# Experts in fixed pairs, each on half of the array's columns

## The chip, the cores and the metric

One core of a Trainium2 chip runs the whole program in one launch. The metric is the device time of a run in microseconds. A profiled execution gives the trace; it has a span (first to last instruction) and a time of its own.

## The reference

Three parts follow one another, all in float32. `_attn_ref`: attention over a window of 128 keys for 4 batches, 8 heads, 576 positions, head size 64. Its output is laid out as 2304 tokens of 512. `_moe_ref`: a mixture of experts over these tokens. `_moe2_ref`: a feed-forward part of width 2048. What matters here is the middle one, with E = 8, D = 512, F = 1024:

```python
do_compute = (x @ w_skip) > 0            # the other tokens stay as they are
xc = x[do_compute]
logits = xc @ w_gate
e_idx = np.argmax(logits, axis=1)
gate_w = softmax(logits)[e_idx]          # per token
for e in range(E):
    mask = e_idx == e
    h = np.maximum(xc[mask] @ w1[e], 0.0)
    y[mask] = gate_w[mask, None] * (h @ w2[e])
out[do_compute] = xc + y
```

Each expert's weights are two matrices of 2 MB. With the inputs as the reference draws them, 1015 of 2304 tokens are computed, and the experts get 102, 111, 174, 146, 175, 133, 94 and 80 of them.

## The kernel before

`program` runs three blocks: `attention`, `experts`, `feed_forward`. A block ends with a barrier of all engines.

**Attention.** 16 pairs of heads (`PAIRS`) are worked off in turn. SP's queue, in the loop over n (L232 to L248), loads v of the next pair, q and k of the one after, one sixteenth of the feed-forward's weights into `ffn["raw"]` (`load_weights`, 512 KB), and stores five tiles of the pair before into the DRAM tensor `tokens`. In `times_values` (L503) the two heads of a pair write partitions 0 to 63 and 64 to 127 of the same PSUM tile.

**Experts.** First the routing, on VectorE with some matmuls. A job is 128 rows of one expert. Each expert has as many jobs as its tokens fill chunks of 128 (L820 to L827), the table says for each job and row which token it holds (`what`, `at_row`, L840 to L846, and the matmuls of L915), and `job_e_i` names the expert of each job. The register `total` is the number of jobs; an engine runs `one(j, slot)` for two jobs and then, in `later_jobs` (L640), under `If`, for those that exist. In a job:

- GpSimd copies the row list (L687), gathers 128 tokens into `x_in` (L691) and, when y is there, scatters it back (L699, L704). A gather of job j + 1 comes behind the scatter of job j - 1.
- PE transposes the tokens (`transpose_x`, L926), multiplies by w1 (`hidden`, L936, two halves c of 512 columns in four steps each; a record in the trace is half of an fp32 matmul, so 16 records), transposes relu(h) (`transpose_h`, L942) and multiplies by w2 (`output`, L952, 16 records).
- VectorE takes relu (L864) and scales y (L885). y lies in the second half of `h_sb`, so relu of the second half waits for the scatter of the job before. ScalarE copies the transposes to SBUF (L742, L750, L757).

SP loads an expert's two matrices into one of two slots when the jobs of the expert two before it are done and the next gather has landed (L666 to L672). In the block's start the first expert is loaded beside the routing. In the first two jobs the weights of the feed-forward are split for the fp32r multiplications: ScalarE copies each of 16 pieces from `raw` to `hi` (L737), VectorE subtracts `lo = raw - hi` (L872); `lo` has the place of `raw`.

**Feed-forward.** Six chunks of 384 tokens in 16 steps f each; its first matmuls wait for all pieces of `lo` (L1264).

`keep_warm` (L73) is a run of matmuls without use in the routing.

Of the kernel before, what the change touches and what calls it, by code (L numbers as in the profile page):

```python
# [8 lines left out]

# [7 lines left out]
F32 = mybir.dt.float32  # L17
F32R = mybir.dt.float32r
I32 = mybir.dt.int32
# [22 lines left out]
FILL = 240  # L42
# [3 lines left out]
CH = N // P  # L46
JOBS = CH + E
# [38 lines left out]
def attention(nc, ctx, dram, ffn, cst):  # L86
# [106 lines left out]
    def _(sp):  # L193
# [23 lines left out]

        def store(n, i):
# [13 lines left out]
        for n in range(PAIRS):  # L232
# [10 lines left out]
            load_weights(n)  # L243
# [297 lines left out]
def experts(nc, ctx, dram, ffn, cst):  # L541
# [9 lines left out]
    w1_sb = sb("w1_sb", [P, 2 * KD * F1])  # L551
    w2_sb = sb("w2_sb", [P, 2 * FB * D])
# [3 lines left out]
    x_in = sb("x_in", [P, 2, D])  # L556
# [3 lines left out]
    used = [FB * D]  # L560

    def scratch(width):
        used[0] += width
        return w2_sb[:, used[0] - width:used[0]]
# [7 lines left out]
    rank, row, weight, number, job1 = (scratch(TT) for _ in range(5))  # L572
# [8 lines left out]
    by_expert = scratch(E * E).rearrange("p (a b) -> p a b", a=E)  # L581
    passed = scratch(JOBS * E).rearrange("p (a b) -> p a b", a=JOBS)
    chunks, ends, first1 = (scratch(E) for _ in range(3))
    job_e = scratch(JOBS)
    count_i = sb("count_i", [P, E], I32)
    ends_i = sb("ends_i", [1, E], I32)
    job_e_i = sb("job_e_i", [1, JOBS + 6], I32)
    table = sb("table", [P, JOBS + 6, 2], I32)
    job_entry = sb("job_entry", [P, 2, 2], I32)
    scatter_list = sb("scatter_list", [P, 2], I32)  # L590
# [19 lines left out]
    w1_loaded = sem("w1_loaded")  # L610
    w2_loaded = sem("w2_loaded")
    entry_copied = sem("entry_copied")
    list_copied = sem("list_copied")
    gathered = sem("gathered")
    xt_ready = sem("xt_ready")
    xt_copied = sem("xt_copied")
    h_ready = sem("h_ready")
    h_relu = sem("h_relu")
    ht_ready = sem("ht_ready")
    ht_copied = sem("ht_copied")  # L620
    y_ready = sem("y_ready")
    y_scaled = sem("y_scaled")
    y_scattered = sem("y_scattered")
    block = ctx.enter_context(nc.Block())

    tables = w1_sb[:, KD * F1:KD * F1 + sum(TABLES.values())]
# [4 lines left out]
    at_row = w1_sb[:, KD * F1 + at:KD * F1 + at + TT * P].rearrange("p (t r) -> p t r", t=TT)  # L631
# [4 lines left out]
    def count_jobs(eng):  # L636
        eng.wait_ge(jobs_ready, 1)
        return eng.value_load(ends_i[0:1, E - 1:E], min_val=E, max_val=JOBS)

    def later_jobs(eng, total, pair, behind=0):  # L640


        with eng.Fori(2, JOBS, 6) as start:
# [5 lines left out]
    def _(sp):  # L649
        sp.dma_start(tables, dram["tables"]).then_inc(tables_loaded, 16)  # L650

        def load_expert(e, slot):
            sp.dma_start(w1_sb[:, slot * KD * F1:(slot + 1) * KD * F1].rearrange("p (k f) -> p k f", k=KD),
                         dram["w1"][e].rearrange("(k p) f -> p k f", p=P)).then_inc(w1_loaded, 16)
            if e:
                sp.wait_ge(w2_loaded, 16 * e)
            sp.dma_start(w2_sb[:, slot * F1 * KD:(slot + 1) * F1 * KD].rearrange("p (k f) -> p k f", f=D),
                         dram["w2"][e].rearrange("(k p) f -> p k f", p=P)).then_inc(w2_loaded, 16)
            sp.wait_ge(w1_loaded, 16 * (e + 1))

        load_expert(0, 0)

        sp.wait_ge(gathered, 32)
        load_expert(1, 1)
        sp.wait_ge(jobs_ready, 1)
        for e in range(2, E):  # L666

            end = sp.value_load(ends_i[0:1, e - 2:e - 1], min_val=1, max_val=JOBS)
            sp.wait_ge(y_ready, end)

            sp.wait_ge(gathered, end * 16 + 32)
            load_expert(e, e % 2)  # L672

    @block.gpsimd
    def _(pool):
        pool.wait_ge(table_ready, 1)
        total = count_jobs(pool)

        def gather(j, slot, later):
            if later:  # L680
                pool.wait_ge(list_copied, j - 1)
                pool.wait_ge(y_scaled, j - 1)
                settled(pool, cst)
            if not isinstance(j, int) or j:
                pool.wait_ge(gathered, j * 16)
                settled(pool, cst)
            nc.gpsimd.tensor_copy(job_entry[:, slot, :], table[:, bass.ds(j, 1), :].rearrange(  # L687
                "p o k -> p (o k)")).then_inc(entry_copied, 1)
            pool.wait_ge(entry_copied, j + 1)
            settled(pool, cst)  # L690
            nc.gpsimd.indirect_dma_start(x_in[:, slot, :], None, dram["x"],  # L691
                                         bass.IndirectOffsetOnAxis(job_entry[:, slot, 0:1], 0),
                                         bounds_check=N + P - 1, oob_is_err=False).then_inc(gathered, 16)

        def scatter(j, slot, later=True):
            if later:
                pool.wait_ge(y_scattered, (j - 1) * 16)
            settled(pool, cst)
            nc.gpsimd.tensor_copy(scatter_list[:, slot:slot + 1], job_entry[:, slot, 0:1]).then_inc(list_copied, 1)  # L699
            pool.wait_ge(list_copied, j + 1)  # L700
            settled(pool, cst)
            pool.wait_ge(y_scaled, j + 1)
            settled(pool, cst)
            nc.gpsimd.indirect_dma_start(dram["x"], bass.IndirectOffsetOnAxis(scatter_list[:, slot:slot + 1], 0),  # L704
                                         y_sb, None, bounds_check=N - 1,
                                         oob_is_err=False).then_inc(y_scattered, 16)


        gather(0, 0, False)
        gather(1, 1, False)  # L710
        scatter(0, 0, False)

        def pair(first):
            with pool.If(first < total):
                gather(first, 0, True)
            with pool.If(first - 1 < total):
                scatter(first - 1, 1)
            with pool.If(first + 1 < total):
                gather(first + 1, 1, True)
            with pool.If(first < total):  # L720
                scatter(first, 0)

        later_jobs(pool, total, pair, behind=1)
        with pool.If(total > JOBS - 1):
            scatter(JOBS - 1, 1)

        pool.wait_ge(y_scattered, total * 16)

    @block.scalar
    def _(act):  # L730
# [3 lines left out]
        act.wait_ge(cst["w_loaded"], 16 * PAIRS)  # L734
        for n in range(PAIRS):
            piece = slice(n * 1024, n * 1024 + 1024)
# [624 lines left out]
```

## Time and profile before

| | us |
|---|---|
| median of three runs | 836.48 (835.88 to 838.04) |
| time of the profiled execution | 835.62 |
| its span | 833.8 |
| attention, up to the routing's first instruction | 178 |
| routing, up to the first transposes of a job | 178 to 202 |
| twelve jobs | 202 to 392 |
| feed-forward, from its first load | 399 to 834 |

The engines' busy times in the span are 796.8 us for PE (96%), 495.9 for VectorE, 367.4 for ScalarE and 357.9 for GpSimd; the mean granted clock of TensorE is 0.99 of full speed. Read a job by the starts on PE's timeline, not by the busy times: the records of a pipelined matmul overlap.

### The profile page before, as it was taken

To read this page: it belongs to the slowest core of one execution; us is meant where nothing else is said; L and a number is where in the kernel's file an instruction comes from. 1 tells how busy PE (TensorE), PEld (TensorE's weight loads), DVE (VectorE), ACT (ScalarE), POOL (GpSimd) and SP (SyncE) were. 2 spreads that over 40 slices of the span, in tenths; PEclk is the share of its full clock that TensorE was granted. 3 is DMA by queue.
4 is the path that set the end of the run, shared out by engine and by line. 5 is a ranking of instruction groups with operands and counts; after the bars stand their busy time and mean duration, and the time that the engine had idled before them with its cause. 6 is when DMAs were issued, how large, how long until landed. Compare 5 with 4: busy or idle time off the path is not lost.

```text
span 833.8 us, 14016 instructions
## 1 busy us (share of the span) xinstructions
PE 796.8 (96%) x4436; PEld 614.5 (74%) x4437; DVE 495.9 (59%) x876; ACT 367.4 (44%) x881; POOL 357.9 (43%) x455
## 2 busy tenths in 40 slices
PE   8999999998999999997599999999999999999996
PEld 4788788876444444443588888888888888988995
DVE  3666666663641111111478877878786887787784
ACT  4677676635110110100355455554555455446453
POOL 3555555301111111111156655655565565655564
PEclk9999999999999999999799999999999999999999
DMA  5656556643584633633200110110100010000001
GB/s 197 190 166 166 165 166 171 164 162 106 216 303 150 243 104 141 240 115 116 75 1 1 39 39 1 38 39 1 39 0 38 0 38 38 0 0 22 18 1 38
DMA packets 50626, 78.07 MB, mean 94 GB/s; under 512 B 22275, under 2 KB 23555, under 8 KB 50560
## 3 DMA queue, kind: packets, MB, share of 16 engines
q1 hardware_dynamic: 48656, 72.20, 26.3%
q0 software_dynamic: 1920, 5.23, 2.0%
q8 instruction: 28, 0.46, 0.2%
q14 instruction: 22, 0.18, 0.1%
HBM read 65.90 MB, written 12.85 MB: 94 GB/s over the span
## 4 chain that ended last, share of the span: by engine, by line
PE 45%; DVE 2%; issue 2%; ACT 1%; POOL 1%; DMA 0%; POOLq 0%; ACTq 0%; DVEq 0%
PE ffn_o L1248 22%; PE ffn_h L1235 22%; DVE n_sb L1206 1%; PE ffn_xt L1223 1%; POOL n_sb L1111 1%; ACT r_sb L1156 1%; DVE u_sb L1189 0%; ACT o_sb L1168 0%; POOL g_lo L1117 0%; DVE u_sb L1198 0%; DVE n_sb L1193 0%; DMA x_sb<-tokens 0%; DVE xt_lo L1180 0%; PE ffn_o L1268 0%; ACT r_sb L1158 0%
## 5 line engine op out<-in xcount | busy, mean ns | idle before, releaser
L1117 POOL TENSOR_TENSOR g_lo<-n_sb,g_hi 128x384 fp32r<-128x384 f32 x96 | 120.0, 1250 | 174.0 <-ACT g_hi L1151 172.0
L1235 PE MATMUL ffn_h<-xt_hi,ffn_lo 128*128 128x384 f32 x384 | 131.4, 342 | 1.9 <-DVE xt_lo L1180 1.9
L1111 POOL TENSOR_TENSOR n_sb<-n_sb,r_sb 128x384 f32<-128x384 f32 x96 | 125.4, 1307 | 18.2 <-DVE r_sb L1200 18.2
L1156 ACT ACTIVATE r_sb<-n_sb,all_consts 128x384 f32<-128x384 f32 x96 | 59.3, 617 | 163.3 <-DVE n_sb L1206 163.3
L1235 PE MATMUL ffn_h<-xt_lo,ffn_hi 128*128 128x384 f32 x384 | 129.7, 338 | 0.0
L1235 PE MATMUL ffn_h<-xt_hi,ffn_hi 128*128 128x384 f32 x384 | 129.1, 336 | 0.0
L1206 DVE SCALAR_TENSOR_TENSOR n_sb<-u_sb 128x384 f32<-128x384 f32 x96 | 124.8, 1300 | 1.8 <-ACT u_sb L1145 1.8
L1248 PE MATMUL ffn_o<-ffn_hi,g_lo 128*128 128x512 f32 x288 | 115.5, 401 | 10.4 <-POOL g_lo L1117 5.3
L1248 PE MATMUL ffn_o<-ffn_hi,g_hi 128*128 128x512 f32 x288 | 113.8, 395 | 0.0
L1248 PE MATMUL ffn_o<-ffn_lo,g_hi 128*128 128x512 f32 x288 | 113.4, 394 | 0.0
L936 PE MATMUL ps_h<-w_sb,x_t 128*128 x192 | 86.3, 603 | 1.1 <-ACT x_t L742 0.9
L1189 DVE TENSOR_SCALAR u_sb<-ffn_h 128x384 f32<-128x384 f32 x96 | 53.2, 554 | 47.2 <-PE ffn_h L1235 47.0
L335 ACT ACTIVATE probs<-ps_scores,neg_max 128x256 f32<-128x256 f32 (+2 forms) x160 | 66.8, 427 | 29.5 <-DVE neg_max L376 29.5
L704 POOL DMA_INDIRECT tokens<-h_sb,scatter_list x12 | 12.2, 1020 | 154.7 <-DVE h_sb L885 154.7
L750 ACT ACTIVATE h_t<-ps_ht 128x512 f32<-128x512 f32 x12 | 7.2, 598 | 159.0 <-PE ps_ht L942 159.0
L1235 PEld LDWEIGHTS ffn_h<-xt_hi,ffn_lo 128*128 128x128 f32 x384 | 72.4, 188 | 5.2 <-DVE xt_lo L1180 2.3
L1235 PEld LDWEIGHTS ffn_h<-xt_lo,ffn_hi 128*128 128x128 f32 x384 | 72.4, 188 | 3.2
L936 PEld LDWEIGHTS ps_h<-w_sb,x_t 128*128 128x128 f32 x192 | 36.9, 194 | 48.4 <-issue 48.4
L1248 PEld LDWEIGHTS ffn_o<-ffn_hi,g_lo 128*128 128x128 f32 x288 | 54.1, 188 | 24.9 <-issue 11.2
L1235 PEld LDWEIGHTS ffn_h<-xt_hi,ffn_hi 128*128 128x128 f32 x384 | 72.3, 188 | 0.0
L1145 ACT ACTIVATE u_sb<-u_sb 128x384 f32<-128x384 f32 x96 | 50.1, 522 | 38.0 <-DVE u_sb L1189 37.8
L376 DVE TENSOR_REDUCE neg_max<-ps_scores 128x2 f32<-128x512 f32 (+2 forms) x80 | 43.6, 578 | 36.5 <-PE ps_scores L475 35.9
(138 smaller groups left out, 1368.4 us busy)
## 6 DMA issues: line engine op xcount, KB each, us to landing
w_sb<-in_w SPq DMA_DIRECT2D x16, 2048.0 KB, 7.9
ffn_raw<-in_w_ffn SPq DMA_DIRECT2D x16, 512.0 KB, 5.3
q_raw<-in_qT SPq DMA_DIRECT2D x16, 288.0 KB, 3.9
k_raw<-in_kT SPq DMA_DIRECT2D x16, 288.0 KB, 4.1
v_sb<-in_v SPq DMA_DIRECT2D x16, 256.0 KB, 2.6
tokens<-x_out SPq DMA_DIRECT2D x64, 64.0 KB, 3.2
x_sb<-tokens SPq DMA_DIRECT2D x5, 768.0 KB, 4.5
out<-o_sb SPq DMA_DIRECT2D x5, 768.0 KB, 3.6
```

The lines of the kernel that those rows point to most:

```text
L335: e = nc.scalar.activation(probs[0:n, r, h, 0:w], ps_scores[t.ring][0:n, h, 0:w], ACT.Exp, bias=neg_max[0:n, r, h:h + 1], scale=-1.0, accu ...
L376: nc.vector.tensor_reduce(neg_max[0:n, r], ps_scores[t.ring][0:n, :, 0:w], AX_X, ALU.min).then_inc(max_ready, 1)
L704: nc.gpsimd.indirect_dma_start(dram["x"], bass.IndirectOffsetOnAxis(scatter_list[:, slot:slot + 1], 0), y_sb, None, bounds_check=N - 1, oo ...
L936: m = t_.matmul(ps_h[c][:, :], x_t[:, k, :], w, start=(k == 0), stop=(k == KD - 1))
L1111: nc.gpsimd.tensor_tensor(n_sb[:, f % NB], n_sb[:, f % NB], r_sb[:, f % 2], ALU.mult).then_inc(ratio_ready, 1)
L1117: nc.gpsimd.tensor_tensor(g_lo[:, f % 2], n_sb[:, f % NB], g_hi[:, f % 2].bitcast(F32), ALU.subtract).then_inc(g_lo_ready, 1)
L1145: nc.scalar.activation(u_sb[:, t.r], u_sb[:, t.r], ACT.Exp).then_inc(u_ready, 1)
L1156: nc.scalar.activation(r_sb[:, t.r], n_sb[:, t.f % NB], ACT.Ln, bias=cst["two"]).then_inc(ln_ready, 1)
L1189: v.tensor_scalar(u_sb[:, t.r], ps_h[t.f % HB][:, 0:C], 20.0, None, ALU.min).then_inc(min_ready, 1)
L1206: v.scalar_tensor_tensor(out=n_sb[:, t.f % NB], in0=u_sb[:, t.r], scalar=2.0, in1=u_sb[:, t.r], op0=ALU.add, op1=ALU.mult).then_inc(n_read ...
L1235: m = nc.tensor.matmul(ps_h[t.f % HB][:, 0:C], ffn[a][:, at:at + P], b[:, t.par, k], start=(n == 0), stop=(n == 3 * KD - 1))
L1248: m = nc.tensor.matmul(ps_o[i][:, :], a[:, t.r, P * i:P * i + P], ffn[b][:, at:at + D], start=(t.f == 0 and n == 0), stop=(t.f == FT - 1 a ...
```

## The change

The eight experts form four fixed pairs (0, 1), (2, 3), (4, 5), (6, 7), worked off in four phases p. A job has 64 rows for each expert of the pair: rows 0 to 63 hold tokens of the even one, rows 64 to 127 of the odd one (`side` adds 64 to the row). A phase has as many jobs as the larger of the two has chunks of 64, at least one. Every matmul of `hidden` and `output` becomes two, with 64 columns of weights each (here the tokens are the stationary operand, the expert's matrix streams), which write partitions 0 to 63 and 64 to 127. The transposes stay as they were. All addresses of weights are fixed in a phase; each engine loads only the number of jobs at its start, and has its own loop for later jobs in each phase.

A pair's weights are 8 MB. Even pairs lie where `hi` will be (`experts_even`), odd ones in `w_sb`, whose space the routing uses before. Pair 0 is loaded in the attention in four loads at n = 6, 8, 10, 12. Pair 1 is loaded when the first gathers have landed, pairs 2 and 3 when the jobs of the pair two before are done; SP doesn't wait for gathers any more. Each phase has semaphores of its own. GpSimd gathers the first two tiles of pair p + 1 before it scatters the first job of pair p; PE transposes the first of them within that job, and ScalarE copies it to `x_first`.

The split of the feed-forward's weights moves: 14 of the 16 pieces are split in the last phase, four of their subtractions on GpSimd; the last two pieces, where `x_in` lies now, are loaded at the feed-forward's start and split in steps 5 and 7 of its first chunk. `FILL` goes from 240 to 216 columns, because the constants have fewer columns.

```diff
-FILL = 240
+FILL = 216
+POOL_PIECES = 4
+LATE = 2
+EARLY = PAIRS - LATE
 TT = B * QT
 GE = E + 1
-CH = N // P
-JOBS = CH + E
+W = P // 2
+PH = E // 2
+PHASE = N // W
+JOBS = PHASE + PH - 1
+LOG_W = W.bit_length() - 1
...
+def pair_weights(dram, buffer, p):
+    first = 2 * KD * F1
+    for half in range(2):
+        yield (buffer[:, half * KD * F1:(half + 1) * KD * F1].rearrange("p (k f) -> p k f", k=KD),
+               dram["w1"][2 * p + half].rearrange("(k p) f -> p k f", p=P))
+    for half in range(2):
+        yield (buffer[:, first + half * KD * F1:first + (half + 1) * KD * F1].rearrange("p (k f) -> p k f", f=D),
+               dram["w2"][2 * p + half].rearrange("(k p) f -> p k f", p=P))
...
+            if n < EARLY:
+                load_weights(n)
+            if n >= HP + 2 and n % 2 == 0 and n < HP + 10:
+                load_experts((n - HP - 2) // 2)
...
-        def load_expert(e, slot):
...
+        def load_experts(p):
+            for i, (to, of) in enumerate(pair_weights(dram, pairs[p % 2], p)):
+                if i == 2:
+                    sp.wait_ge(w1_loaded[p], 32)
+                sp.dma_start(to, of).then_inc(w1_loaded[p] if i < 2 else w2_loaded[p], 16)
+        sp.wait_ge(first_gathered, 1)
+        load_experts(1)
         sp.wait_ge(jobs_ready, 1)
-        for e in range(2, E):
-            end = sp.value_load(ends_i[0:1, e - 2:e - 1], min_val=1, max_val=JOBS)
-            sp.wait_ge(y_ready, end)
-            sp.wait_ge(gathered, end * 16 + 32)
-            load_expert(e, e % 2)
+        for p in range(2, PH):
+            done = jobs_of(sp, p - 2)
+            sp.wait_ge(y_ready[p - 2], done)
+            settled(sp, cst)
+            load_experts(p)
...
+        def gather_two(p):
+            total = jobs_of(pool, p)
+            first = pool.value_load(jobs_i[0:1, PH + p:PH + p + 1], min_val=0, max_val=JOBS - 1) if p else 0
+            gather(p, 0, 0, first)
+            with pool.If(total > 1):
+                gather(p, 1, 1, first)
+                if p == 0:
+                    pool.wait_ge(gathered[0], 32)
+            if p == 0:
+                pool.wait_ge(gathered[0], 16)
+                pool.sem_inc(first_gathered, 1)
+            return total, first
+        def low_parts():
+            for n in range(POOL_PIECES):
+                piece = slice(n * 1024, n * 1024 + 1024)
+                pool.wait_ge(cst["w_hi_ready"], n + 1)
+                nc.gpsimd.tensor_tensor(ffn["lo"][:, piece], ffn["raw"][:, piece], ffn["hi"][:, piece].bitcast(F32),
+                                        ALU.subtract).then_inc(cst["w_lo_by_pool"], 1)
...
+        ahead, before = gather_two(0), None
+        for p in range(PH):
+            total, first = ahead
+            if p < PH - 1:
+                ahead = gather_two(p + 1)
+            else:
+                low_parts()
+            scatter(p, 0, 0, before)
...
+            if p == PH - 1:
+                act.wait_ge(cst["w_loaded"], 16 * EARLY)
+                act.wait_ge(y_ready[p - 1], before)
+                high_parts(range(7))
+            one_now = functools.partial(one, p, total=total)
+            one_now(0, 0)
+            if p == PH - 1:
+                high_parts(range(7, EARLY))
...
+        then(v.tensor_tensor(in_job[:, :, 0:E], onehot, over_t(cst["odd"]), ALU.mult))
+        then(v.tensor_reduce(side, in_job[:, :, 0:E], AX_X, ALU.add))
...
+            split = p == PH - 1 and isinstance(i, int) and i == 0
+            relu(p, i, 0, before)
+            if split:
+                low_parts(range(4, 5))
+            relu(p, i, 1, before)
+            if split:
+                low_parts(range(5, 11))
+            scale_y(p, i, slot)
+            if split:
+                low_parts(range(11, 13))
...
-                m = t_.matmul(ps_h[c][:, :], x_t[:, k, :], w, start=(k == 0), stop=(k == KD - 1))
...
+        def hidden(p, i, c):
+            x = x_t
+            if isinstance(i, int) and i == 0:
+                x = x_first
+                if c == 0:
+                    pe.wait_ge(first_copied, p + 1)
+                    pe.wait_ge(w1_loaded[p], 32)
+            elif c == 0:
+                pe.wait_ge(xt_copied[p], i)
+            for k in range(KD):
+                for side in range(2):
+                    mine = slice(W * side, W * side + W)
+                    m = t_.matmul(ps_h[c][mine, :], x[:, k, mine], weights(p, 0, side, k * F1 + c * half),
+                                  start=(k == 0), stop=(k == KD - 1))
+            m.then_inc(h_ready[p], 1)
...
+        def one(p, i, slot, total, done_before=None):
+            hidden(p, i, 0)
+            hidden(p, i, 1)
+            transpose_h(p, i, 0)
+            with pe.If(i + 1 < total):
+                transpose_x(p, i + 1, 1 - slot)
+            if isinstance(i, int) and i == 0 and p < PH - 1:
+                transpose_first(p + 1)
+            transpose_h(p, i, 1)
+            if not isinstance(i, int):
+                pe.wait_ge(y_scaled[p], i - 1)
+            elif i == 0 and p:
+                pe.wait_ge(y_scaled[p - 1], done_before)
+            output(p, i, slot, 0)
+            output(p, i, slot, 1)
...
+        for n in range(EARLY, PAIRS):
+            sp.dma_start(ffn["raw"][:, n * 1024:n * 1024 + 1024], dram["w_ffn"][n]).then_inc(cst["w_loaded"], 16)
...
+            if isinstance(c, int) and c == 0 and f in SPLIT:
+                piece = slice(SPLIT[f] * 1024, SPLIT[f] * 1024 + 1024)
+                act.wait_ge(cst["w_loaded"], 16 * PAIRS)
+                nc.scalar.activation(ffn["hi"][:, piece], ffn["raw"][:, piece],
+                                     ACT.Copy).then_inc(cst["w_hi_ready"], 1)
...
+            if isinstance(t.c, int) and t.c == 0 and t.f == FT - 2 * LATE:
+                pe.wait_ge(cst["w_lo_ready"], PAIRS - POOL_PIECES)
...
+        ffn["pair"] = nc.alloc_sbuf_tensor_at("experts_even", [P, 4 * KD * F1], F32, offset=ffn["free"])
+        ffn["late"] = at_lo + EARLY * 1024 * 4
```

`output` is split like `hidden`, `scatter` and `gather` only take the phase beside the job, and `relu` waits for the scatter before it also across two phases.

## Rows read from the trace of the kernel before

**Rows 1.** Windows: length, PE, PEld, DVE, ACT, POOL busy, clock, DMA share, GB/s.

```profile
280.00:320.00 40.00, 39.83 (x111) 18.76 (x110) 5.71 (x8) 3.37 (x6) 7.38 (x12) 1.00 0.58 210
...
418.00:421.00 3.00, 3.00 (x12) 2.56 (x11) 2.65 (x4) 1.20 (x4) 2.00 (x2) 0.51 0.00 0
```

**Rows 2.** Timeline of PE, jobs of the expert stage, first feed-forward `output`.

```profile
236.93 7.13 PE L936 MATMUL ps_h<-w_sb,x_t 128*128 x16
243.90 0.60 PE L942 MATMUL ps_ht<-all_consts,h_sb 128*128 128x128 f32 x4
244.33 0.61 PE L926 MATMUL ps_xt<-all_consts,x_in 128*128 128x128 f32 x4
244.94 0.66 PE L942 MATMUL ps_ht<-all_consts,h_sb 128*128 128x128 f32 x4
245.44 3.60 PE L952 MATMUL ps_y<-w_sb,h_t 128*128 x8
...
252.31 7.03 PE L936 MATMUL ps_h<-w_sb,x_t 128*128 x16
...
360.46 7.03 PE L936 MATMUL ps_h<-w_sb,x_t 128*128 x16
...
416.62 0.47 PE L1248 MATMUL ffn_o<-ffn_hi,g_lo 128*128 128x512 f32 x1 [1.89 <-POOL g_lo L1117]
```

**Rows 3.** Timeline of SP's queue, loads of experts 3 and 4.

```profile
244.26 0.38 SPq L653 DMA_DIRECT2D w_sb<-in_w  x1
...
275.53 0.37 SPq L653 DMA_DIRECT2D w_sb<-in_w  x1
```

**Rows 4.** Timeline of PE in the attention; last, line 503 (ns min/median/max).

```profile
110.90 0.22 PE L475 MATMUL ps_scores<-k_hi,q_lo 64*64 64x64 f32 x2
110.95 0.22 PE L475 MATMUL ps_scores<-k_hi,q_hi 64*64 64x64 f32 x2
...
111.50 1.09 PE L503 MATMUL ps_out_t<-probs_t,v_sb 128*64 128x128 f32 x16
112.52 0.76 PE L514 MATMUL ps_x<-back_gate,out_t 128*128 128x146 f32 x4
...
L503 PE MATMUL ps_out_t<-probs_t,v_sb x40: 272/273/324, 99.8 to 112.0; 128*64 128x128 f32 x40
```

**Rows 5.** Groups of instructions by line, routing on DVE (busy us, mean ns).

```profile
L840 DVE TENSOR_TENSOR w_sb<-all_consts,w_sb 128x104 f32<-128x104 f32 x3 | 0.8, 258 | 0.0
...
L851 DVE TENSOR_TENSOR w_sb<-all_consts,w_sb 128x208 f32<-128x208 f32 x1 | 0.4, 369 | 0.0
```

**Rows 6.** Timeline of GpSimd and PE around a gather; last, L638, its register load (ns).

```profile
254.33 1.03 POOL L704 DMA_INDIRECT tokens<-h_sb,scatter_list  x1 [12.38 <-DVE h_sb L885]
...
256.44 1.04 POOL L691 DMA_INDIRECT x_in<-tokens,job_entry  x1 [0.89 <-POOL job_entry L687]
...
260.08 0.66 PE L926 MATMUL ps_xt<-all_consts,x_in 128*128 128x128 f32 x4 [0.31 <-DMA x_in<-tokens,job_entry]
...
L638 POOLq TENSOR_LOAD <-ends_i x1: 500/500/500, 195.7 to 195.7; - x1
...
L638 POOLq FUSED_REGOPS  x1: 190/190/190, 196.3 to 196.3; - x1
```

**Rows 7.** Windows, attention and expert stage, one microsecond each.

```profile
83.00:84.00 1.00, 1.00 (x20) 0.85 (x16) 0.69 (x2) 0.31 (x3) 1.00 (x1) 1.00 0.00 0
...
247.00:248.00 1.00, 1.00 (x3) 0.38 (x2) 0.00 (x0) 0.00 (x0) 0.00 (x0) 1.00 1.10 442
```

**Rows 8.** Timeline of the split of w_ffn; lines 265 and 1206 (ns min/median/max).

```profile
182.98 15.24 ACT L737 ACTIVATE ffn_hi<-ffn_raw 128x1024 fp32r<-128x1024 f32 x16
...
212.57 9.16 DVE L872 TENSOR_TENSOR ffn_lo<-ffn_raw,ffn_hi 128x1024 fp32r<-128x1024 f32 x8
...
L265 POOL TENSOR_TENSOR q_lo<-q_raw,q_hi x12: 1412/1415/1430, 43.0 to 153.3; 128x576 fp32r<-128x576 f32 x12
...
L1206 DVE SCALAR_TENSOR_TENSOR n_sb<-u_sb x96: 551/1368/1399, 409.7 to 820.3; 128x384 f32<-128x384 f32 x96
```

More of the change, by code:

```diff
@@ L550, in experts @@
     FB = F1 // P
-    w1_sb = sb("w1_sb", [P, 2 * KD * F1])
-    w2_sb = sb("w2_sb", [P, 2 * FB * D])
+    w_sb = sb("w_sb", [P, 4 * KD * F1])
+    pairs = (ffn["pair"], w_sb)
     h_sb = sb("h_sb", [P, F1])
@@ L571, in experts @@
     top, chosen, expsum = scratch(TT), scratch(TT), scratch(TT)
-    rank, row, weight, number, job1 = (scratch(TT) for _ in range(5))
+    rank, row, weight, number, job1, side = (scratch(TT) for _ in range(6))
     pad = 16
@@ L709, in _ @@
[L709 to L725, printed above, removed]
@@ new lines, in _, with pair @@
+        for p in range(PH):
[5 more added lines that the diff above has]
+            scatter(p, 0, 0, before)
+            def pair(i):
+                with pool.If(i < total):
+                    gather(p, i, 0, first)
+                with pool.If(i - 1 < total):
+                    scatter(p, i - 1, 1)
+                with pool.If(i + 1 < total):
+                    gather(p, i + 1, 1, first)
+                with pool.If(i < total):
+                    scatter(p, i, 0)
+            later_jobs(pool, total, pair, behind=1)
+            before = total
@@ L729, in _ @@
+        pool.wait_ge(y_scattered[PH - 1], before * 16)
     @block.scalar
@@ L831, in _ @@
-        then(v.scalar_tensor_tensor(out=first1, in0=ends, scalar=1.0, in1=chunks, op0=ALU.add, op1=ALU.subtract))
-        v.tensor_tensor(number, number, row, ALU.subtract)
-        then(v.tensor_tensor(work, onehot, over_t(first1), ALU.mult))
+        then(v.tensor_copy(chunks, count_i[:].rearrange("p (a b) -> p a b", a=PH)))
+        v.tensor_tensor(row, row, side, ALU.add)
+        then(v.tensor_reduce(jobs, chunks, AX_X, ALU.max))
+        then(v.tensor_scalar(jobs, jobs, 1.0, None, ALU.max))
@@ L889, in _, with relu @@
-        one(0, 0)
-        one(1, 1)
-        def pair(first):
-            for slot in range(2):
-                with dve.If(first + slot < total):
-                    one(first + slot, slot)
-        later_jobs(dve, total, pair)
+        def relu(p, i, c, before):
+            dve.wait_ge(h_ready[p], i * 2 + c + 1)
+            if c == 1:
+                if not isinstance(i, int) or i:
+                    dve.wait_ge(y_scattered[p], i * 16)
+                elif p:
+                    dve.wait_ge(y_scattered[p - 1], before * 16)
+            v.tensor_scalar(h_sb[:, half * c:half * c + half], ps_h[c][:, :], 0.0, None, ALU.max).then_inc(h_relu[p], 1)
@@ new lines, in weights @@
+        def weights(p, layer, side, at):
+            start = (2 * layer + side) * KD * F1 + at
+            return pairs[p % 2][:, start:start + half]
+        def hidden(p, i, c):
[13 more added lines that the diff above has]
+            m.then_inc(h_ready[p], 1)
@@ new lines, in _, with pair @@
+        transpose_first(0)
+        pe.wait_ge(jobs_ready, 1)
+        done_before = None
+        for p in range(PH):
+            total = jobs_of(pe, p)
+            one(p, 0, 0, total, done_before)
+            with pe.If(total > 1):
+                one(p, 1, 1, total)
+            def pair(i):
+                for slot in range(2):
+                    with pe.If(i + slot < total):
+                        one(p, i + slot, slot, total)
+            later_jobs(pe, total, pair)
+            done_before = total
```

368 lines of the change are left out of this document (181 added, 187 removed).

## The prediction

> **What bounds the kernel now.** Read the page's first two parts first: TensorE (PE) is busy 96% of the span at a granted clock of 0.99, so only work that PE no longer does, or no longer waits for, shortens the kernel. The change is in the expert stage, so the windows of that stage come next: from 280 to 320 us PE is busy 39.83 of 40 us while VectorE has 5.71, ScalarE 3.37, GpSimd 7.38 and the DMA engines are busy 0.58 [rows 1]. PE alone is full there. Then the timeline of PE inside one job: 16 records of `hidden` 6.97 us (from 236.93 to 243.90), four transposes of h 0.43, four of the next x 0.61 with a short wait, four of h 0.50, 16 records of `output` 6.87 [rows 2]. Seven jobs from 252.31 to 360.46 take 15.45 us each [rows 2]. Of that, 13.7 us are the 32 streams of 512 columns at 6.87/16 = 0.429 us. A job is paid in full whether its 128 rows hold tokens or not, so the number of jobs and the price of a job are the two things to work out.
>
> **The number of jobs.** The router's counts, worked out from the reference's inputs, are 102, 111, 174, 146, 175, 133, 94 and 80 tokens for the eight experts. In chunks of 128 this is 1, 1, 2, 2, 2, 2, 1, 1 = 12 jobs, as the trace has them: the load for expert 3 is issued at 244.26 and that for expert 4 at 275.53, two jobs later [rows 3]. A pair now takes as many jobs as its larger expert has chunks of 64: (102, 111) 2, (174, 146) 3, (175, 133) 3, (94, 80) 2, in sum 10. Two jobs fewer at 15.45 are **-30.9 us**, if a job costs what it did.
>
> **The price of a job.** Each 128x512 stream becomes two streams of 128x64 weights, one per half of the columns, so the job keeps its time only if the two halves run at once. The kernel already does this in `times_values` of the attention, where two heads write partitions 0 to 63 and 64 to 127 of ps_out_t. Sixteen such records of 128 columns take from 111.50 to 112.52 [rows 4]. A full-width fp32 record of 128 columns takes 0.43/4 = 0.1075 us [rows 2], so one after the other they would need 1.72; they took 1.02. They run in pairs: the last starts at 111.50 + 1.09 - 0.272 = 112.32 (0.272 is the duration of one), so eight pairs are (0.82)/7 = 0.117 apart, 0.01 more than one full-width record [rows 4]. Is that 0.01 fixed or a share of 9%? The row halves in `scores` come every 0.05 us with 64 columns (110.90 to 110.95), twice their share of streaming, which looks like a fixed amount per pair [rows 4]. I take it as fixed: 32 pairs x 10 jobs x 0.01 = 3.2 us. From the last pair to the next kind of matmul 0.20 us pass, 0.09 more than a stream [rows 4]; a job changes between half and full width twice: 10 x 2 x 0.09 = 1.8. Together **+5.0**; bounds 0 (the extra time hidden under 512 columns) and 14 (9% of 137 us, and the 1.8).
>
> Here the Trainium skill speaks against the change: "TensorE: Matmul & The Clock Gate", section "Measured speedup vs the span model", has three column tiles with 512 columns at 2.38x instead of 3x. By that, as an estimate, a pair would cost about 0.54 us and the kernel would end near 855 us. The rows of this trace stand nearer to 2x for a run of pairs; the sum goes by them, and the page's case is the second rival below.
>
> **The routing.** Two dependent instructions of 160 elements come in for `side`, the small instructions are roughly exchanged, and the five rounds that make `what` have 39 jobs instead of 26, so three instructions of 156 elements instead of 104. 104 elements take 258 ns and 208 take 369 [rows 5]: 52 more are 0.056 us, 15 times 0.8. The two for `side` are 0.32 each by the same slope, and I let nearly all of it count: **+1.5**, bounds 0.8 and 2.5. Everything behind it is a chain (table, list, gather, first transposes), so it counts.
>
> **The start of a pair.** The gather of the next pair's first tile is issued by GpSimd only when the loop of the pair before is left; PE asks for it in the middle of the pair's first job (`transpose_first`). Count from the first `hidden` of a job, 252.31. GpSimd's scatter instruction of the job before runs from 2.02 to 3.05 and now, 1.08 later, the gather from 4.13 to 5.17; the transposes that wait for it start at 7.77 (260.08, 0.31 idle), 2.6 after the instruction's end [rows 6]. An expert load was in flight then (issued at 244.26, with the DMA engines full from 247 to 248 [rows 3, 7]), so a load beside it does not add much. In the changed kernel GpSimd first runs through six empty or half empty turns of the loop (about 2 us from the end of the scatter's issue at 2.0, an estimate; branches are not on the critical path now), then loads two registers at 0.50 + 0.19 each [rows 6]: free at 5.4 instead of about 3. The copy and the gap are 1.1, the instruction 1.04, the landing 2.6: 10.1. PE wants it after `hidden` (7.1 at the new price), 0.43 and 0.49 of transposes: 8.05. So about 2.1 us late, at pairs 1 and 2; in the first job of pair 0 the cold start of PE hides it. **+4.2**; bounds 0 and 8. What is queued behind it on PE is the second half's transposes and the whole `output`; on GpSimd the scatter of that job, not due before 16. An idle PE of 1.89 us at 416.62 was followed by a granted clock of 0.51 for three microseconds [rows 1, 2], which cost 1.5; I charge this for one of the two stalls: **+1.5**, bounds 0 and 3. PE's own loops at the three changes of pair run ahead of its queue for the most part; entering the loop at 236.93 cost 0.1 now (6.97 against 6.87) [rows 2]. I take 0.3 each, **+0.9**, bounds 0 and 2. Job 0 transposes one tile more: **+0.4**.
>
> **The weights.** 8 MB for pair 0 move into the attention, four loads of 2 MB, one in every second pair of heads from n = 6. Each comes behind q, k, v and the piece of w_ffn in SP's queue, and the five stores and the next q, k and v queue behind it. At 442 GB/s [rows 7] 2 MB are 4.7 us; in the attention the engines stand still between two pairs of heads (share 0.00 from 83 to 84 us [rows 7]), so I price it at 0. If that cover were gone, every load would delay the next q and k by up to 5 us. Pairs 1 to 3 each need 8 MB (at the rate of the window, some 20 us) and have 31 or 46 us of jobs to land under: 0. Behind SP's waits for them (first_gathered, the y of the pair before last, the first layer landed) stand only later weight loads. The two pieces of w_ffn that come later are needed only at step 12 of the feed-forward's first chunk.
>
> **The split of w_ffn.** Sixteen ScalarE copies of 0.95 (15.24 in all) and sixteen VectorE subtractions of 1.15 (9.16 for eight) lay under the first two jobs [rows 8]. Now 14 of the copies, 10 subtractions on VectorE and four on GpSimd lie under the two jobs of the last pair, because the pair weights occupy the space of `hi`. GpSimd takes 1.415 us for 576 columns [rows 8], so about 2.5 for 1024, 10 for four, and it does them before it scatters the job: free at about 15, when the job's y is due. VectorE with both operands in SBUF is slower while GpSimd works: the same instruction takes from 0.55 to 1.37 [rows 8]. Four of its subtractions fall into GpSimd's time at up to 2.8 each, so it reaches the scaling of y some 2 us late; the scatter follows, and relu of the next job waits for the scatter: **+2.3**, bounds 0 and 6. Two copies and two subtractions lie in the first chunk of the feed-forward: **+1.0**, bounds 0 and 4. The tail, scatter to first feed-forward transposes, is the same.
>
> **Sum.** -30.9 + 5.0 + 1.5 + 4.2 + 1.5 + 0.9 + 0.4 + 2.3 + 1.0 = -14.1. The profiled execution took 835.62, so 821.5; the median of the runs is 0.86 above it: 822.
>
> **The rivals.** (1) The two halves run one after the other: 10 x 13.7 more, 835.6 - 30.9 + 137 + 12 = about 954. Against it stand 1.02 us for what would take 1.72 [rows 4]. 4 in 100. (2) They overlap, but a pair of long streams is slower by a share: at the 1.72/1.02 = 1.69 of the whole attention block a pair takes 0.508, 320 pairs cost 25 us more, and the kernel ends at 842, slower than before. It decides from 0.48 us per pair on. The spacing of 0.117 speaks against it. 8 in 100. The Trainium skill's page named above speaks for it. (3) GpSimd becomes the bound at each change of pair, and the split of w_ffn collides: with the upper bounds of these terms (8, 3, 6, 4 and 2) the gain shrinks to under 4 us, 832 to 838. 8 in 100. (4) The gather is in time and the split hides: -30.9 + 5.0 + 1.5 + 0.4 and 1 for the rest, 813. 15 in 100. That the change does not cut the jobs is excluded by the counts. My own forecast, 816 to 830, has 65 in 100.
>
> **Range and chances.** Leaving out the slow ends of (1) and (2) and little on the fast side: 808 to 836. Faster by over 0.3% (2.5 us, about what a measurement of this kernel can tell from no change) 0.82, within it 0.06, slower 0.12; cases (4), the forecast and a part of (3) make up the first, the rest of (3) the second, (1), (2) the third.
>
> **What would show it.** Half-width records in pairs about 0.44 us apart and jobs of about 15.7; ten `h` scalings; a wait of PE for a gather near 8 us into the first jobs of pairs 1 and 2; GpSimd subtractions under the last pair, with VectorE's beside them longer than 1.15; attention windows as full as now. Wrong would be: pairs 0.5 or more apart, q or k late in the attention, or PE waiting for pair weights.

## The result, and the profile after

The changed kernel takes 849.47 us (847.62 to 851.36, four runs) against 836.18 for the kernel before: 1.0155 times, with a 95% interval of 1.0125 to 1.0186. It is slower, where 822 was forecast. The profiled execution took 848.45 with a span of 846.7, 12.9 more than before. The ratios further down leave out two executions that were over 1.5% longer than the fastest of their kernel (838.05 in e6, 842.68 in e10); the medians include them. By the starts on PE's timelines, stage by stage (the last output's end is its start plus 3.43, the spacing of two output halves):

| stage | before | after | difference | forecast |
|---|---|---|---|---|
| up to the first transposes of a job | 201.58 | 204.25 | +2.7 | +1.5 |
| jobs, to the last output's end | 189.94 | 187.40 | -2.5 | -16.6 |
| tail, to the first feed-forward transposes | 9.85 | 12.85 | +3.0 | 0 |
| from these to the first `hidden` of the feed-forward | 4.77 | 5.56 | +0.8 | 0 |
| from there to the end | 427.66 | 436.64 | +9.0 | +1.0 |

Ten jobs run, and a job that nothing disturbs costs nearly what it did. Before, a first layer (`hidden`) of 16 full-width records that doesn't stand behind the start of the loop took 6.86 us:

```profile
283.36 7.03 PE L936 MATMUL ps_h<-w_sb,x_t 128*128 x16
290.22 0.60 PE L942 MATMUL ps_ht<-all_consts,h_sb 128*128 128x128 f32 x4
```

PE's timeline after the change (start, duration, then line and tiles, idle time before it in brackets) shows a first layer of 32 half-width records from 226.65 to 233.62, 6.97 us, so 0.11 more:

```profile
204.25 0.71 PE L1010 MATMUL ps_xt<-all_consts,x_in 128*128 128x128 f32 x4 [2.23 <-DMA x_in<-tokens,job_entry]
205.64 10.00 PE L1037 MATMUL ps_h<-experts_even,x_first 128*64 128x512 f32 x32 [0.69 <-ACT x_first L800]
...
226.65 7.04 PE L1037 MATMUL ps_h<-experts_even,x_t 128*64 128x512 f32 x32
233.62 0.66 PE L1044 MATMUL ps_ht<-all_consts,h_sb 128*128 128x128 f32 x4
...
240.12 3.60 PE L1055 MATMUL ps_y<-experts_even,h_sb 128*64 128x512 f32 x16
248.39 8.78 PE L1037 MATMUL ps_h<-w_sb,x_first 128*64 128x512 f32 x32 [4.67 <-issue]
...
304.93 9.85 PE L1037 MATMUL ps_h<-experts_even,x_first 128*64 128x512 f32 x32 [3.38 <-issue]
...
359.05 8.40 PE L1037 MATMUL ps_h<-w_sb,x_first 128*64 128x512 f32 x32 [3.44 <-issue]
```

The loss stands in the brackets. At each of the three changes of pair PE is idle with "issue" as the reason: it waits for no semaphore, its own sequencer has nothing to hand it. These are 4.67 + 3.38 + 3.44 = 11.5 us, and the layers behind them run partly at the lower of TensorE's two clocks, 1.2 instead of 2.4 GHz (durations of 8.78, 9.85 and 8.40 instead of 7.04). The windows say the same (length, PE's busy time, then PEld, DVE, ACT, POOL, the granted clock, the DMA share and GB/s): the last one is the start of the layer behind the second gap, with a granted clock of 0.50. Before, PE was busy 39.83 of 40 us at clock 1.00 [rows 1]:

```profile
240.00:280.00 40.00, 32.70 (x148) 12.98 (x146) 4.27 (x6) 3.96 (x7) 6.11 (x10) 0.91 0.66 242
280.00:320.00 40.00, 36.31 (x166) 13.13 (x164) 4.27 (x6) 3.29 (x6) 4.88 (x8) 0.91 0.42 150
...
304.90:308.00 3.10, 3.07 (x8) 1.12 (x10) 0.00 (x0) 0.00 (x0) 0.00 (x0) 0.50 1.00 395
```

What the sequencer does there is on the lines of `later_jobs`: L681 the outer loop over later jobs in steps of six, L682 its condition, L683 the inner loop. Rows by line (times in ns, min/median/max, then the first and last start):

```profile
L681 PEldq COMPARE_BRANCH  x24: 76/214/247, 243.4 to 391.8; - x24
L682 PEldq COMPARE_BRANCH  x24: 77/221/3742, 239.5 to 391.5; - x24
L682 PEldq COMPARE_BRANCH  x1: 3742/3742/3742, 239.5 to 239.5; - x1
L682 POOLq COMPARE_BRANCH  x24: 39/50/50, 228.5 to 399.3; - x24
```

24 is six turns in each of four pairs, though no pair has work for more than one. A branch costs PE's sequencer 0.21 to 0.22 us in the median, and an empty outer turn 0.76. The loop of the first pair begins at 239.3, while the outputs still run to 243.72, and ends at 247.2: PE's queue covers the first four microseconds of it and no more. At this first change one long branch, the 3.74 us at 239.5, takes up that cover, and the five turns behind it and the load of the next pair's number of jobs stand in the open. At the other two changes no branch is that long, and the empty turns of the outer loop, with those of the inner one ahead of them, outlast the queue by themselves. On GpSimd the same turns last in the tail from 396.6 to 399.6; the loads of the first feed-forward tiles follow at 401.81.

In the feed-forward the two late split steps stand in VectorE's chain, here with an idle of 2.19 for ScalarE's copy and 1.2 of its own, twice:

```profile
434.45 1.37 DVE L1323 SCALAR_TENSOR_TENSOR n_sb<-u_sb 128x384 f32<-128x384 f32 x1
438.02 1.22 DVE L1332 TENSOR_TENSOR ffn_lo<-ffn_raw,ffn_hi 128x1024 fp32r<-128x1024 f32 x1 [2.19 <-ACT ffn_hi L1277]
...
450.12 1.23 DVE L1332 TENSOR_TENSOR ffn_lo<-ffn_raw,ffn_hi 128x1024 fp32r<-128x1024 f32 x1 [2.19 <-ACT ffn_hi L1277]
```

So the theory (A): the gain of two jobs went to empty loop turns on the sequencers and to the late split. The rivals: the idle at a change of pair is something else that happens there, such as fetching code or waiting for weights (B), and the feed-forward loses by its late, slow start, not by the split.

### The profile page after: what moved, and what is told of

Read it like the earlier page. It is cut to its first block, busy times and chain, and to the rows that moved or that the text cites. A ratio compares the mean times of both kernels' runs of the same rounds, so it can differ in the third digit from the quotient of the medians.

```text
span 846.7 us, 14478 instructions
## 1 busy us (share of the span) xinstructions
PE 784.0 (93%) x4668; PEld 591.6 (70%) x4668; DVE 494.1 (58%) x868; ACT 364.3 (43%) x875; POOL 365.0 (43%) x451
## 3 DMA queue, kind: packets, MB, share of 16 engines
q1 hardware_dynamic: 48656, 72.19, 25.7%
## 4 chain that ended last, share of the span: by engine, by line
PE 41%; DVE 4%; issue 3%; ACT 2%; POOL 1%; DMA 1%; POOLq 0%; SPq 0%; ACTq 0%; DVEq 0%
PE ffn_o L1373 20%; PE ffn_h L1358 20%; DVE n_sb L1323 2%; ACT r_sb L1268 1%; POOL n_sb L1223 1%; PE ffn_xt L1346 1%; DVE u_sb L1306 1%; DVE u_sb L1315 1%; POOL g_lo L1229 1%; DVE n_sb L1310 1%; DMA x_sb<-tokens 1%; ACT o_sb L1285 0%; ACT r_sb L1270 0%; DVE xt_lo L1297 0%; ACT ffn_hi L1277 0%
## 5 line engine op out<-in xcount | busy, mean ns | idle before, releaser
L1373 PEld LDWEIGHTS ffn_o<-ffn_hi,g_lo 128*128 128x128 f32 x288 | 54.3, 189 | 29.3 <-issue 14.2
L1373 PEld LDWEIGHTS ffn_o<-ffn_hi,g_hi 128*128 128x128 f32 x288 | 54.2, 188 | 13.3
L940 DVE TENSOR_SCALAR h_sb<-ps_h 128x512 f32<-128x512 f32 x20 | 13.8, 691 | 79.6 <-PE ps_h L1037 67.0
L1373 PEld LDWEIGHTS ffn_o<-ffn_lo,g_hi 128*128 128x128 f32 x288 | 54.2, 188 | 8.5
```

The costliest lines, as they stand in the source:

```text
L940: v.tensor_scalar(h_sb[:, half * c:half * c + half], ps_h[c][:, :], 0.0, None, ALU.max).then_inc(h_relu[p], 1)
L1373: m = nc.tensor.matmul(ps_o[i][:, :], a[:, t.r, P * i:P * i + P], ffn[b][:, at:at + D], start=(t.f == 0 and n == 0), stop=(t.f == FT - 1 a ...
```

## The experiments

Ratios are to the kernel before, run on the same chip; differences in microseconds are of ratios times 836.5. The loop with one turn allows a pair 8 jobs instead of 38, of which these inputs need 3.

**One turn (e1).**

```diff
-        with eng.Fori(2, PHASE + 2, 6) as start:
+        with eng.Fori(2, 8, 6) as start:
```

> The outer loop over later jobs has one turn instead of six on every engine, so a pair can have at most 8 jobs instead of 38; these inputs need 3 at most. Theory A (the empty turns on the sequencers eat the gain): PE's idle at the three changes of pair falls from 4.7, 3.4 and 3.4 us to about 1 or nothing, the first layer behind them runs at 6.97 instead of 8.3 to 9.8, GpSimd leaves its loop some 3 us earlier in the tail: 849 - 10 - 5 - 3 - 2 (gathers) = about 828. Rival B (PE fetches code or waits for weights at a change of pair, the loop's length means nothing): the idle of 3.4 to 4.7 us stays, 847 to 850.

Measured: 846.27, ratio 1.0107 (1.0052 to 1.0162), only 4 us less, and the interval overlaps that of the change. The idle of the changes of pair is gone, and the tail is back at 9.87. But PE now stands still a few microseconds later:

```profile
246.64 7.09 PE L1037 MATMUL ps_h<-w_sb,x_first 128*64 128x512 f32 x32 [0.16 <-issue]
...
260.31 1.11 PE L1010 MATMUL ps_xt<-all_consts,x_in 128*128 128x128 f32 x4 [5.56 <-DMA x_in<-tokens,job_entry]
261.22 1.06 PE L1044 MATMUL ps_ht<-all_consts,h_sb 128*128 128x128 f32 x4
262.21 5.11 PE L1055 MATMUL ps_y<-w_sb,h_t 128*64 128x512 f32 x16
...
302.44 7.04 PE L1037 MATMUL ps_h<-experts_even,x_first 128*64 128x512 f32 x32
...
316.40 1.12 PE L1010 MATMUL ps_xt<-all_consts,x_in 128*128 128x128 f32 x4 [5.90 <-DMA x_in<-tokens,job_entry]
```

A is right on the place and the mechanism, wrong on the sum: the turns had covered another wait, the gather of the next pair's first tile, that takes 5.56 and 5.90 us and the lower clock behind them (a granted clock of 0.50 from 262 to 265, and a duration of 5.11 for an output half of 3.65). The step the other way, twelve turns instead of six (e2, expected at about 866), has no measured time, so no run has more than six turns.

**Early split (e3).** The copies and subtractions of both late pieces go ahead of the first step (VectorE's side of the edit):

```diff
             xt_part(0, 0, k, first_xt[k])
+        for n in range(EARLY, PAIRS):
+            piece = slice(n * 1024, n * 1024 + 1024)
+            dve.wait_ge(cst["w_hi_ready"], n + 1)
+            v.tensor_tensor(ffn["lo"][:, piece], ffn["raw"][:, piece], ffn["hi"][:, piece].bitcast(F32),
+                            ALU.subtract).then_inc(cst["w_lo_ready"], 1)
         run_steps(dve, step, 2)
```

> The two late pieces of the feed-forward's weights are split ahead of its first step instead of in steps 5 and 7 of its first chunk. Theory A: VectorE's two waits for ScalarE's copy inside the chain of steps go, and with them about 7 us: 842. Rival B (the loss in the feed-forward is its late start and the cold clock of its first matmuls, not the split): 848 to 850.

Measured: 842.64, 1.0081 (1.005 to 1.0111), 6 us less than the change: the split inside the chain was the larger part of the feed-forward's 9 us. The last stage of the table falls from 436.6 to 431.2 in the profiled execution, against 427.7 before. The other 3.5 us stay, here and in all later runs (431.3 in e9). By the starts of VectorE's steps, 1.1 of them are there after the first five steps: the first matmuls of the feed-forward run at a granted clock of 0.50 (408.6 to 414 in e3), where the kernel before had 1.00 (406 to 412), so rival B has a part too. The rest comes evenly, some 0.4 us in each later chunk, and its cause is open.

**Both (e4).**

> One turn, and the split ahead of the first step. Theory A: the two gains add, about 821, faster than the kernel before by 1.8%. Rival B: 845 to 850.

Measured: 839.35, 1.003 (1.0006 to 1.0053), 10.5 us less than the change; so 4.0 and 6.2 add up, within the noise. Most of the 18 us that are missing are PE's two stalls for the gather, here 5.12 and 5.78, and the lower clock behind them.

**Transposes of the next pair's tile at the job's end (e5)**, with e4's edits:

```diff
             transpose_h(p, i, 0)
+            if isinstance(i, int) and i == 1 and p < PH - 1:
+                pe.wait_ge(first_copied, p + 2)
...
-            if isinstance(i, int) and i == 0 and p < PH - 1:
-                transpose_first(p + 1)
             transpose_h(p, i, 1)
...
             output(p, i, slot, 1)
+            if isinstance(i, int) and i == 0 and p < PH - 1:
+                transpose_first(p + 1)
```

> One turn, the early split, and the transposes of the next pair's first tile (with ScalarE's copy of them) moved from the middle of a pair's first job to behind its outputs. With one turn PE stood still 5.6 and 5.9 us for that tile's gather and then ran at half clock, some 15 us in sum; the gather had landed 13.7 us after the start of the job, the new place comes at 15. Theory A2 (the gather is the next stall in line, and was covered by the empty turns before): 839 - 15 = 824, 12 us under the kernel before. Rival C (the stall moves on: to the second gather, the scatter, the weights): 833 to 840.

Measured: 830.36, 0.992 (0.9904 to 0.9935). The two stalls are gone; of the 15 us, 6 came back, most of them as waits of 3.40 and 2.19 for the gather of a third tile and smaller ones for the scatter. Both theories have a part.

**Load behind the gather (e6)**, with e4's edits:

```diff
             sp.wait_ge(y_ready[p - 2], done)
             settled(sp, cst)
+            sp.wait_ge(gathered[p], 16)
             load_experts(p)
```

> One turn, the early split, transposes where they were; SyncE issues the next 8 MB of pair weights only when the first gather of that pair has landed. Theory D (the gather is slow because the 8 MB fill the DMA queues): it lands 2.6 us after its instruction instead of 6.0, PE's two stalls shrink from 5.6 and 5.9 to about 2, 839 - 7 = 832. Rival (GpSimd's late start alone; the load costs nothing): stalls as they were, 839.

Measured: 829.87, 0.9889 (0.9853 to 0.9926), 12 us less than e4 by the ratios, 9 by the medians; D holds. First GpSimd in e4, where the 8 MB are issued at 246.93, then in e6, where they are issued at 256.63. The gather's instruction begins 0.2 us apart in the two; the next copy, which waits for its landing, comes 6.02 us behind its end in the one and 2.58 in the other:

```profile
253.45 1.05 POOL L722 DMA_INDIRECT x_in<-tokens,job_entry  x1 [0.93 <-POOL job_entry L718]
260.52 0.18 POOL L718 COPY job_entry<-table 128x2 int32 x1 [6.02 <-DMA x_in<-tokens,job_entry]
```

```profile
253.24 1.05 POOL L723 DMA_INDIRECT x_in<-tokens,job_entry  x1 [0.93 <-POOL job_entry L719]
256.88 0.19 POOL L719 COPY job_entry<-table 128x2 int32 x1 [2.58 <-DMA x_in<-tokens,job_entry]
```

PE's two stalls shrink to 1.27 and 2.50, and behind them the matmuls keep their full-clock durations (3.65 for an output half).

**Six turns again (e7)**, on e5.

> The kernel with the early split and the late transposes, but with six outer turns again: what the turns cost where nothing else waits beside them. Theory A: PE's idle of 4.7, 3.4 and 3.4 us comes back with the half clock behind it (16 to 18) and the tail's 3: 19 to 21 above the kernel with one turn, about 844. Rival B (the idle at a change of pair is something else): within 4 us of the kernel with one turn.

Measured: 837.41, 1.0006 (0.9991 to 1.002), 7 us above e5, where 19 to 21 were expected. The idle is back (4.02, 3.38 and 3.37), but the two waits for a third tile (3.40, 2.19) shrink to nothing and 0.22: part of what the turns cost is again time in which PE would have waited.

**All four edits (e9).** One turn, early split, late transposes, late load.

> One turn, early split, late transposes, and the pair's load behind its first gather. Late transposes and late load each took 9 us off the kernel with one turn and early split (839 to 830); what is left of waits for a gather (3.4 and 2.2 us for a third tile with late transposes) came with the load beside it. Theory: the two edits cover mostly the same stall and the second removes the rest, 826. Rival (they are one and the same): 830.

Measured: 822.91, 0.9858 (0.9838 to 0.9878), 1.4% faster than the kernel before. The two cures of the gather are not the same thing.

**Six turns on PE alone (e11)**, on e9.

> The kernel with one turn, with six turns on PE alone; the other engines keep one. Theory A (each engine pays for its own turns): PE's idle of 3.4 to 4.7 us is back at the three changes of pair, the tail stays at 9.9 us: 826 + 11 + 5 = about 840, less what the idle covers of other waits. Rival E (PE stood still because another engine's turns were late): no idle, 826.

Measured: 840.86, 1.0058 (1.0035 to 1.0081), 16.7 us above e9: with little left to cover, the turns cost nearly what was put on them at first. Not all of it is theirs: in the profiled execution, the slowest of eleven, 4.1 us arose in the routing, where the granted clock was 0.50 from 191.5 to 204 against 1.00 in e9, and 19.0 in the jobs. The tail is no part of it (9.92). The profile has the idle at the three changes of pair, the first longer than in any other run; there the first branch of L682 took 6.04 us instead of 3.74:

```profile
247.28 9.62 PE L1038 MATMUL ps_h<-w_sb,x_first 128*64 128x512 f32 x32 [6.82 <-issue]
...
L682 PEldq COMPARE_BRANCH  x24: 77/221/6042, 236.2 to 396.3; - x24
```

**One turn and a guard (e10)**, on e9, with all 38 jobs possible:

```diff
+        turns(2, 8)
+        with eng.If(total > 8 - behind):
+            turns(8, PHASE + 2)
```

> The same, but with all 38 jobs for each pair again: one turn, and the five others behind one more condition that is false here. Theory A: a false condition costs one branch (0.2 us) on each engine, within 2 us of the kernel with one turn, 826 to 828. Rival (the size of the program between two pairs costs time in itself): 5 us or more above it.

Measured: 835.83, 0.9995 (0.9971 to 1.0019), 11.5 us above e9 (in the profiled executions 14.2 in the jobs and 3.8 in the routing): the rival is right. The condition is false and no turn behind it runs; yet PE's idle is back (4.40, 2.86 and 2.41). The jump over the second copy of the loop's code takes PE 2.76, 3.33, 0.34 and 2.71 us behind the four pairs. At the first change the first false branch inside the loop comes on top, with 4.68. At the third the jump is short, and 2.5 us pass instead between two register instructions of the next pair's start. The guard's line on PE and on ScalarE, the two register instructions, then PE's timeline at the first change:

```profile
L688 PEldq COMPARE_BRANCH  x4: 339/2738/3333, 244.1 to 388.1; - x4
L688 ACTq COMPARE_BRANCH  x4: 45/48/50, 237.1 to 385.0; - x4
...
L676 PEldq FUSED_REGOPS  x1: 158/158/158, 356.0 to 356.0; - x1
L676 PEldq SEQ_ASSERT  x1: 18/18/18, 358.7 to 358.7; - x1
...
247.77 9.68 PE L1043 MATMUL ps_h<-w_sb,x_first 128*64 128x512 f32 x32 [4.40 <-issue]
```

So B isn't false everywhere: in the changed kernel the idle is the turns at the second and third change, and at the first the turns together with one long branch; and more code between two pairs can make an idle of the same size without any turn. The Trainium skill ("Runtime: NRT & Kernel Launch", section "Instruction fetch mechanics") says that a taken branch whose target isn't loaded has to wait for a DMA fetch; the 2.74 us in the median agree with it, though no run here separates the fetch from the rest of the branch, and the stall at the third change is on no branch's row.

**Loop to the pair's own number of jobs (e12)**, with the other three edits:

```diff
-        with eng.Fori(2, PHASE + 2, 6) as start:
+        with eng.Fori(2, total + behind if behind else total, 6) as start:
```

> The kernel with all four edits (the loop's edit, early split, late transposes, late load), where the loop over later jobs ends at the pair's own number of jobs, read from the register, instead of after one turn: all 38 jobs for each pair are possible again, no empty outer turn is worked through and no code is jumped over that the one-turn kernel doesn't jump over. If empty turns and far jumps are what cost: as the one-turn kernel, 823 to 825. Rival (a loop bound in a register costs as much as the guard): 830 or more.

Measured: 824.36, 0.9872 (0.9849 to 0.9895). All 38 jobs are possible again, and the time is that of e9 within the noise.

**Warm-up in the routing (e8 on e5, e13 on e12):** `keep_warm(nc, ps_y[0], cst, 13)` instead of 10 ahead of the table.

> One turn, early split, late transposes, and three more warm-up matmuls on PE ahead of the routing's table (13 instead of 10). If the 2.7 us of the routing are partly PE's clock: the wait of 1.86 ahead of the table matmuls falls to 0.7, the second eight of them take 1.0 instead of 1.8, 1.5 to 2 us off, about 822.5. If VectorE's longer instructions alone set the rounds: no change, 824.

> The same, and three more warm-up matmuls on PE ahead of the routing's table. If the clock in the routing is worth something in most executions: 821 to 823 and a smaller spread; if VectorE alone sets the rounds: as without it.

Measured: e8 828.77, 0.9917 (0.99 to 0.9935), as e5; e13 821.75, 0.9835 (0.9812 to 0.9859), the fastest of all, but its interval overlaps that of e12. In both, the wait of 1.85 ahead of the table fell to 0.76. Without the edit the clock in the table's five rounds differs between kernels that are the same up to there: eight matmuls take 1.12 in all rounds of e9 and 1.83 in four of e11, whose first job begins 4.1 us later. In e8 and e13 they take 1.12. Whether the three warm-ups are worth something in the median is open. The windows of e13 over the first changes of pair, where PE is now busy 38 of 40 us at a granted clock of 1.00:

```profile
240.00:280.00 40.00, 38.09 (x186) 14.53 (x188) 5.48 (x8) 3.86 (x7) 7.34 (x12) 1.00 0.68 248
280.00:320.00 40.00, 38.21 (x190) 14.59 (x188) 4.96 (x7) 5.05 (x9) 6.11 (x10) 1.00 0.48 173
```

## Why the prediction was wrong

**The step that failed** is the one sentence on loops: "PE's own loops at the three changes of pair run ahead of its queue for the most part … I take 0.3 each", 0.9 in sum with an upper bound of 2. The three changes took 11.5 us of idle and, by the layers behind the three gaps against 6.97 (8.72, 9.78 and 8.33, start to start), another 5.9 at a lower clock. The price came from entering the loop once, with work in it, at 0.1 [rows 2]; the kernel before has one such loop for all jobs, in which the empty turns come once, after the last job, beside the tail's other waits. The change has four loops, three of them in PE's path. The trace before has the price of an empty turn, but the prediction didn't use it. It counted six empty or half empty turns on GpSimd, at about 2 us, and none on PE. In that trace the loop (L643, its condition L644) makes four outer turns, and the last two are empty. On PE they end 0.75 us apart, while the last outputs run to 391.5 and cover them:

```profile
L643 PEldq COMPARE_BRANCH  x3: 76/214/214, 387.4 to 388.9; - x3
L644 PEldq COMPARE_BRANCH  x2: 214/214/214, 387.8 to 388.5; - x2
```

Five or six such turns at 0.75 are some 4 us at each change of pair (an estimate from these rows), as much as the queue's whole cover in the trace after. The first change has the long branch of L682 besides, 3.74 us, which no row of before shows. It is no matter of the number of turns: it takes 3.3 to 4.4 us in the runs with one turn too, where PE's outputs cover most of it (0.16 idle in e1, 1.20 in e12).

**The same turns in the tail.** "The tail … is the same" was worth 3.0: the barrier waits for GpSimd, which leaves its last loop 3 us later. Without these turns the tail is 9.87 in e1 and 9.66 in e9.

**The split in the feed-forward**, +1.0 with an upper bound of 4, was mis-sized: 6 us by e3. The durations were nearly right (1.04 and 1.22 after, 0.95 and 1.15 before [rows 8]); what was left out is that the subtraction waits in VectorE's queue for a copy that itself waits in ScalarE's chain. So each of the two steps takes VectorE 3.4 us (2.19 idle, 1.22 busy), and ScalarE, behind its copy, waits 1.76 for VectorE. Another 3.5 us of the stage, described at e3, are no term of the sum.

**The gather** was the right worry at the wrong price. "A load beside it does not add much" failed: before, SP issued an expert's load only when the next gather had landed, and the change took that wait away; now the pair's 8 MB and the gather of the pair's first tile are set off by the same event, the end of a pair. Landing takes 6.0 us instead of 2.6 (e4 and e6). In the changed kernel this was nearly invisible (0.75 idle at 258.95), since PE came late itself; with the turns away it cost some 7.5 us at each of two pairs (5.56 and 5.90 idle, the rest lower clock), not 2.1.

**Right:** the number of jobs; the attention's loads at next to no cost (the routing's first matmul is at 178.55, before at 178.25; the other profiles lie between 177.58 in e5 and 179.19 in e13); the split in the last pair, where the subtractions on VectorE beside GpSimd took up to 3.05 and PE waited 0.64. The +5.0 for pairs of half-width streams came out at about 1.5: a `hidden` takes 6.97 against 6.86, an `output` 6.91 (236.64 to 243.55) against 6.87 [rows 2], so 0.15 a job. Rivals 1 and 2 are out. The Trainium skill ("TensorE: Matmul & The Clock Gate", section "Measured speedup vs the span model") has three column tiles at 2.38 times the rate of one instead of 3; the two halves here run at 1.97 times the rate of one. The routing's +1.5 was right as well: from its first matmul to the first transposes it takes 25.7 us against 23.3 before, but 24.5 and 24.6 in the profiles of e9 and e13, where the clock is up in all rounds. So 1.2 are the longer instructions, and the rest is the clock.

With the turns, the split and the gather mended the kernel takes 822 to 824. That this is the forecast's 822 is partly chance: the halves cost 3.5 less than put down, and waits for the scatter and the third tile and the feed-forward's 3.5, which weren't put down, stand in their place.

**Left open:** why the first branch of L682 at the first change of pair takes 3.3 to 4.4 us in every run with this line, and 6.0 in e11 (the DMA engines were full beside it there, 1.00 to 1.05 from 234 to 240, and idle in the changed kernel, so load alone doesn't make it long); why the feed-forward's first matmuls run at the lower clock and each of its later chunks takes some 0.4 us longer; and the spread of 11 to 13 us between executions of e6, e10 and e11, against 2 for e9; the clock in the routing can make up some 4 us of it.

## What to carry to other kernels

When a change turns one loop into several, count what each engine's sequencer does when there is no work: turns times branches, on PE at 0.2 us each, against the few microseconds of work that its queue holds; end the loop at the number in the register, and beware of large unused code between two phases. When a wait is taken away, ask what it kept apart: the load that used to wait for the gather now collides with it. And when a stall is mended and the time hardly moves, look for the next wait on the same engine before dropping the theory: here three causes hid one another, and only together were they worth some 25 us.

## What the hardware showed that was not expected

- A COMPARE_BRANCH takes PE's sequencer 0.21 to 0.22 us in the median, GpSimd's 0.05 and ScalarE's 0.05. The Trainium skill ("Advanced Engine Details and Errata", section "Control Flow Timing") has one figure of about 108 ns and names no engine; PE's is twice that here, the others' half.
- A jump over code that doesn't run took PE 2.74 us in the median of four in e10 (0.34 to 3.33), ScalarE 0.05 on the same line.
- A gather of 128 rows of 2 KB lands 2.6 us after its instruction alone (e6) and 6.0 beside an 8 MB load on SP's queue (e4).
- Two 64-column halves of the array, 512 columns streamed through each, run almost fully side by side: 32 records in 6.97 us, against 6.86 for 16 full-width ones.
